# Block-causal attention ahead of two feed-forward stages: one inversion of the row sums per head, attention pipeline one to two steps deeper

## The reference

```
scores = q @ k.T / 8
scores = where(i // 64 >= j // 64, scores, -1e9)
attn = exp(scores - rowmax)
attn = attn / (attn.sum(-1) + 1e-9)
x = attn @ v                                  # 2304 x 512 after the heads are joined
x = (sigmoid(x @ w_gate) * (x @ w_val)) @ w_out      # 512 -> 1536 -> 512
p = domain_probs / (domain_probs.sum(-1) + 1e-9)
out = sum over 4 experts e of  p[:, e] * (relu(x @ w1[e]) @ w2[e])   # 512 -> 1024 -> 512
```

## Time and profile before

| | |
|---|---|
| Time, three runs | 1467.77, 1469.93, 1473.21 us (median 1469.93) |
| Profiled execution: its own time | 1468.38 us |
| its span | 1466.6 us |
| Busy over the span | PE 97%, PEld 88%, DVE 62%, ACT 50%, POOL 29% |
| Mean granted TensorE clock | 0.995 of full |

### The profile page before, as it was taken

One profiled execution on the slowest core, in us unless ns is written; L12 is line 12 of the kernel. 1 busy time (PEld: TensorE's weight loads), 2 busy tenths in 40 slices (PEclk: granted clock), 3 DMA queues, 4 the chain that ended last, 5 costly groups with the idle time before them and its releaser, 6 DMA issues.

```text
span 1466.6 us, 22252 instructions
## 1 busy us (share of the span) xinstructions
PE 1418.0 (97%) x7816; PEld 1288.6 (88%) x7816; DVE 905.8 (62%) x1557; ACT 728.5 (50%) x1472; POOL 424.0 (29%) x665
## 2 busy tenths in 40 slices
PE   6999988899999999999999999999999999999999
PEld 4777776799998989898999989899899999899897
DVE  4888879777646446376774546364857746364453
ACT  4878777666434334254663534253546535253341
POOL 3656655544302122021441112021134312021200
PEclk9999999999999999999999999999999999999999
DMA  7787797223214121122223132131222322131302
GB/s 177 182 205 179 188 225 174 60 66 87 81 35 144 44 86 59 57 87 86 65 81 100 60 100 65 51 95 45 77 87 72 98 61 72 44 101 43 97 12 79
DMA packets 201150, 136.76 MB, mean 93 GB/s; under 512 B 66096, under 2 KB 170576, under 8 KB 201040
## 3 DMA queue, kind: packets, MB, share of 16 engines
q1 hardware_dynamic: 200976, 135.31, 33.2%
q0 software_dynamic: 64, 0.04, 0.1%
HBM read 97.55 MB, written 9.44 MB: 73 GB/s over the span
## 4 chain that ended last, share of the span: by engine, by line
PE 84%; DVE 8%; DMA 2%; issue 2%; ACT 1%; SPq 1%; POOL 1%; ACTq 0%; DVEq 0%; POOLq 0%
PE pb L903 26%; PE pb L905 25%; PE pb L904 25%; PE pt L395 3%; PE ov L420 2%; DVE ptl L330 2%; DVE nmax L308 1%; PE st L432 1%; PE st L383 1%; DMA craw<-in_moe_w_dram 1%; PE st L384 1%; DVE x1p L343 1%; DMA xb<-x1d 1%; DVE qtl L336 1%; DVE ktl L336 1%
## 5 line engine op out<-in xcount | busy, mean ns | idle before, releaser
L903 PE MATMUL pb<-xch,ul 128*128 128x384 f32 x1176 | 398.9, 339 | 5.7 <-DVE cb L837 4.2
L905 PE MATMUL pb<-xch,uh 128*128 128x384 f32 x1176 | 393.5, 335 | 0.0
L904 PE MATMUL pb<-xcl,uh 128*128 128x384 f32 x1176 | 393.3, 334 | 0.0
L697 POOL TENSOR_TENSOR us<-ura 128x256 f32<-128x256 f32 x84 | 62.3, 742 | 851.4 <-DVE ul L659 833.2
L903 PEld LDWEIGHTS pb<-xch,ul 128*128 128x128 f32 x1176 | 220.7, 188 | 23.8 <-issue 16.7
L905 PE MATMUL pb<-ch,rh 128*128 128x512 f32 x576 | 224.6, 390 | 0.0
L904 PE MATMUL pb<-cl,rh 128*128 128x512 f32 x576 | 224.5, 390 | 0.0
L903 PE MATMUL pb<-ch,rl 128*128 128x512 f32 x576 | 224.0, 389 | 0.0
L904 PEld LDWEIGHTS pb<-xcl,uh 128*128 128x128 f32 x1176 | 220.9, 188 | 0.4
L905 PEld LDWEIGHTS pb<-xch,uh 128*128 128x128 f32 x1176 | 220.7, 188 | 0.0
L806 DVE TENSOR_TENSOR cl<-craw,ch 128x512 fp32r<-128x512 f32 x132 | 92.0, 710 | 114.4 <-ACT ch L741 114.0
(11 more groups left out here) (99 smaller groups left out, 2558.2 us busy)
## 6 DMA issues: line engine op xcount, KB each, us to landing
ura<-in_moe_w_dram SPq DMA_DIRECT2D x96, 256.0 KB, 3.1
craw<-in_moe_w_dram SPq DMA_DIRECT2D x96, 256.0 KB, 2.8
ura<-in_moe_w_gate_dram SPq DMA_DIRECT2D x36, 256.0 KB, 3.2
ura<-in_moe_w_val_dram SPq DMA_DIRECT2D x36, 256.0 KB, 3.2
craw<-in_moe_w_out_dram SPq DMA_DIRECT2D x36, 256.0 KB, 3.1
qhl<-qth SPq DMA_DIRECT2D x32, 144.0 KB, 2.7
qhl<-qtl SPq DMA_DIRECT2D x32, 144.0 KB, 2.6
qlh<-qtl SPq DMA_DIRECT2D x32, 144.0 KB, 2.6
```

The source lines that it names most:

```text
L697: nc.gpsimd.tensor_tensor(us[:, 0, :], a21, a22, ALU.add).then_inc(us_ok, 1)
L903: nc.tensor.matmul(acc, lhs[1], rhs[0], start=start, stop=False, skip_group_check=True)
L904: nc.tensor.matmul(acc, lhs[0], rhs[1], start=False, stop=False, skip_group_check=True)
L905: return nc.tensor.matmul(acc, lhs[0], rhs[0], start=False, stop=stop, skip_group_check=True)
```

## The change

The row sums of a head are completed and inverted once, after its fifth tile, instead of after the third and again after the fifth. Since the first tiles of a head can be normalised only then, the transpositions and the halves of them come two steps later (LAG_T 6 to 8, LAG_HI 5 to 7, LAG_LO 6 to 8), and the product with v and the output one step later (LAG_PV 13 to 14, LAG_OHI 15 to 16, LAG_OLO 16 to 17). The loop gets one more step at its end (TAIL), and from p5(1) on the products woven in at the end stand one step later.

```diff
--- before.py
+++ after.py
@@ -25,7 +25,7 @@
 
 
 STEPS = 5 * HEADS
-TAIL = 17
+TAIL = 18
 X1_RING = 2
 
 
@@ -56,9 +56,9 @@
     MASKED = -1e30
     SCALE = 1.0 / D ** 0.5
 
-    LAG_T, LAG_HI, LAG_LO, LAG_PV, LAG_OHI, LAG_OLO = 6, 5, 6, 13, 15, 16
+    LAG_T, LAG_HI, LAG_LO, LAG_PV, LAG_OHI, LAG_OLO = 8, 7, 8, 14, 16, 17
     PV_PARTS = {0: (0,), 1: (1,), 2: (2, 3, 4)}
-    INVERSE = {0: 3, 3: 5}
+    INVERSE = {0: 5}
     BODY = 20
 
     AT = [0, 256, 512, 896, 1408]
@@ -1152,18 +1152,18 @@
                 p7(0)
             if k == 6:
                 p1(1)
-            if k == 7:
+            if k == 8:
 
                 pe.wait_ge(pt_lo, 6 * HEADS)
                 p5(1)
-            if k == 8:
+            if k == 9:
                 p4(0)
                 p6(1)
-            if k == 9:
+            if k == 10:
                 p2(1)
-            if k == 10:
+            if k == 11:
                 p3(1)
-            if k == 11:
+            if k == 12:
                 p7(1)
 
         attention(nc, block, q, k, v, x1d, o_ok, x1_out, with_act, with_dve, with_pool, with_pe, with_sp)
```

## The result

The changed kernel takes 1520.95 us (median of 4 runs, 1518.31 to 1523.18), the kernel before 1471.07 beside it (1467.77 to 1473.21): 1.0342 times as long, 95% interval 1.0326 to 1.0358. That is 49.9 us more. The forecast was 31 more, 1500, in a range that ended at 1516: the sign was right and the size was not.

A forecast was written before the change was run, and what follows sets the result against it. Attention was taken as bound by a loop handed round between engines, 7.66 us a head. Terms 37 + 1 - 1 - 10 + 4 gave +31 us, so 1500 us, with an 8-in-10 range of 1481 to 1516.

The forecast's parts named there:

- loop, 26 heads: Attention, fourth head to last that makes a prep: 9.08 us a head against 7.66, +37 us.
- two heads without prep: Attention's two heads without a prep: 8.1 us against about 7.5, +1 us (0 to 3).
- side work and clock: Attention: side work partly falls into VectorE's new gaps and the `xb` wait shrinks, -10 us (-20 to 0).
- filling: Pipeline start: for two more steps TensorE has no transpositions ahead of its scores, -1 us (-3 to 0).
- end: Attention's end: leftover TensorE work and p5(1)'s wait for VectorE's last split cost together +4 us (1 to 6).
- A: From tile 0's row maximum to tile 2's: TensorE's list sets it, 3.25 us, between 3.10 and 3.4.
- B: From tile 2's row maximum to tile 3's: VectorE's work with tile 4 and the output, 2.00 us (before 0.74).
- C: From tile 3's row maximum to the next head's tile 0: same road as before, 3.83 us against 3.76.
- third rival: Attention loop: only VectorE's lists count, TensorE keeps ahead; loop 8.2 us, total 1480 us; chance 10%.
- The saving: VectorE, between tiles 3 and 4: removed completion and inversion, up to 0.46 us a head, counted at 0 (-15 to 0).
- GpSimd: Its five normalisations now in a row, later ones each needed a step later: 0 us (0 to 3).
- a rival, at 8%: Attention: TensorE's gaps lower the clock; if in every second head, +20 us, total 1520 us; chance 8%.

The follow-up runs named there:

- mends: Changed kernel with unread filler transpositions in TensorE's two waits, mixing weights in step 44 not 40, VectorE's unit 2 weight splits behind head 30's output sum: 1503.7 us.
- the tail edit: Changed kernel with VectorE's two splits of unit 2's weights at k = 8 instead of k = 7, behind the output sum of head 30: 1514.8 us.
- The experiment that moved the pair: Kernel before, with VectorE's completion and inversion for tiles 0 to 2 behind the row maximum of tile 4 instead of ahead of it: 1475.33 us.
- The kernel with earlier products: Changed kernel with product with v and output a step earlier (LAG_PV, LAG_OHI, LAG_OLO = 13, 15, 16): 1537.89 us.

## Why the prediction was right in its loop and too low in its sum

The middle is 26 heads with a prep and two without. In us of the profiled executions (the last column is the changed kernel with the three edits together, here called mends, span 1502.5; its M0 at 41.98 and 307.95):

| term | forecast | measured | with the mends |
|---|---|---|---|
| loop, 26 heads: 9.11 - 7.66 each | +37 | +37.7 | +37.7 |
| two heads without prep: 8.37 - 7.59 each, by the undisturbed one | +1 | +1.6 | +1.6 |
| side work and clock: the rest of the middle | -10 | +3.9 | -9.5 |
| filling | -1 | +3.95 | +2.6 |
| end | +4 | +6.05 | +3.5 |
| sum | +31 | +53.2 | +35.9 |

Of the 22.2 us that the sum is short, 13.9 are side work and clock, 4.95 filling, 2 the end and 1.3 the loop with the two heads.

**The loop: right.** Forecast 3.25 + 2.00 + 3.83 = 9.08; measured 3.36 + 2.11 + 3.63 = 9.10. The signs named for it are there: two gaps in VectorE instead of one (0.87 and 1.51, where some 0.8 and 2 were named), TensorE's wait for the split of tile 4, its wait for exp ahead of prep. That the sum is right to 0.02 is luck: A and B were 0.11 longer each and C 0.20 shorter. The bounds stated for this term, 34 to 43, do not follow from the ends of A either; 3.10 and 3.4 give 33 and 41. (The third rival's terms, too, make 1484 and not 1480.) One sign of being wrong came too, in the profile of the tail edit only: a granted clock under 1 in heads without side work. That two steps cost so much and one step about 0.55 shows what a lag is in a loop of five: not only a depth, but a place in each engine's list.

**The saving: right at 0.** The experiment that moved the pair, and the one that kept both inversions in the deep pipeline, show it from two sides. VectorE's 85% was no reason to count it.

**GpSimd: right at 0 in the quiet loop, and by a narrow margin.** At a lag of 6 the single inversion makes TensorE wait 45.7 us for it; at 7 the matmuls wait 5.1 us and at 8 (the changed kernel) 1.6, the weight loads ahead of them still 18.8.

**Side work: this step failed.** I took 10 us off since side work would fall into the loop's new gaps. The last column shows that it does, when the clock stays: -9.5. But side work that lands on VectorE or ScalarE also adds to TensorE's waits, and the clock fell. Six times in attention that happened, each for one to two heads, and it took back the whole credit and 4 us more. I had the fall as a rival, at 8%, and had put it aside by one row, where TensorE was busy 2.87 of 4 us and kept its clock. That row is like the quiet loop here (14.26 of 18.30 busy is 3.1 of 4, and the clock did hold), not like the heads with side work, where TensorE was busy 1.80 of 4 us ahead of the fall. The price of a fall could be read in the first row of that group (a clock of 0.63); what I had not asked is how many more there would be: six in the middle where before had two. The Trainium skill's page "TensorE: Matmul & The Clock Gate" says in "A second HAM failure mode: psum-queue depth-cycling" that frequent short pauses between groups of matmuls can make the clock swing and that the loss comes between the bursts. This trace agrees in kind: no wait of TensorE ahead of the fall at 96 was longer than 1.69 us. The quiet loop's pauses of 1.14 and 0.82 us in each head left the clock at 1.00 for 36 us (52 to 88) here, and in the profile of the tail edit it fell behind such pauses (105.60).

So the rival had the mechanism that the forecast lacked, and not its form. In this profile the falls stand in or just behind heads with side work, not in every second head. They don't come at fixed places, though: the profile of the tail edit has two of its falls in heads without any. What starts a fall stays open; that removing the step-40 job or filling the waits makes most of them go is what the runs show. The rival's sum (+20, 1520) agrees with the measured time partly by luck, because filling and end, which it took as forecast, were short by 7 us as well.

**The filling: this step failed too.** Forecast -1, measured +4.0. Five prep matmuls take 1.39 us at 27.6 and 1.41 still at 40.1; before they took 1.26 at 28.0 and 0.83 at 36.9. So the changed kernel's TensorE was still at 1.2 GHz at about 41 us, where before it had left that level by 37 us. That it has fewer transpositions to do there is a likely reason, not a tested one. With the mends, where the prep at 28.1 takes 0.86 and the one at 39.7 takes 0.91, it is still +2.6; what of the +3.95 is the clock and what the order was not separated.

**The end: near, with one term missing.** The +1.5 for `p5(1)` is the first row of TensorE's waits here, 1.28. The second I had not seen (TensorE's waits in its timeline):

```profile
346.11 0.44 PE L903 MATMUL pb<-xch,ul 128*128 128x384 f32 x1 [1.28 <-DVE ptl L330]
349.96 0.66 PE L420 MATMUL ov<-pth,vs 128*128 128x384 f32 x1 [2.54 <-DVE x1p L343]
```

VectorE's timeline shows what the output sum stood behind:

```profile
345.97 0.68 DVE L651 TENSOR_TENSOR ul<-ura,uh 128x512 fp32r<-128x512 f32 x1
347.80 1.23 DVE L659 TENSOR_TENSOR ul<-us,uh 128x1024 fp32r<-128x1024 f32 x1 [1.15 <-ACT uh L639]
349.06 0.76 DVE L343 TENSOR_TENSOR x1p<-ov,x1p 64x576 f32<-64x576 f32 x1
```

With the later lags the sum of head 30 comes behind the weight splits of the second unit, which wait 1.15 us for ScalarE. The clock is 0.71 in the window from 348 to 352. With the splits in another order the end is +3.5, near the forecast of +4.

So 18.9 us were missed between the medians (49.9 for 31). With the mends the kernel is 34.3 us above the kernel before beside it, so they take back 15.6, and what they leave is the forecast within 4 us. That side work and lost clock together made the loss in the middle is shown: with the waits filled and the step-40 job moved, 13.4 us of it go, and so do five of the six falls. How much of it is wait and how much is clock is not told apart, since each causes the other.

## What to carry to other kernels

- In a software pipeline over engines that work their lists in order, a lag also fixes where in the cycle an instruction stands. Lay out the two or three lists that hand the loop round, with start-to-start times, before adding a lag: that gave each of three parts within 0.2 us here and their sum, 9.10, within 0.02, while busy shares gave nothing.
- When a loop gets gaps in TensorE, price falls of the clock as a term of their own, first for the iterations where something else adds a wait, and take no credit for side work that "falls into the gaps" unless the clock holds there.
- One profile shows where the clock fell in one execution. A second execution of the same lists had as much clock lost, 20.4 us, at other places, so compare the sum and not a single fall.

## What the runs showed of the hardware

- Matmuls that nobody reads can keep the clock up: with 14 transpositions per head where TensorE waits, 6.9 us of clock are lost from 44 us on instead of 22.2. The quiet loop is 9.11 us as without, and the kernel 8.7 us shorter.
- The waits of one head do not tell whether the clock falls. The quiet loop, with gaps of 1.14 and 0.82 us in 9.1, kept a granted clock of 1.00 from 52 to 88 us in one profile. Behind waits of 1.69, 1.14 and 0.86 us it fell to 0.51 in that profile (100 to 104). In the profile of the tail edit the same three waits left it at 1.00, and it fell to 0.70 (104 to 108) and 0.50 (116 to 120) in heads with the quiet loop's waits alone. The kernel with earlier products, whose waits of 0.81 and 1.14 us stand 1.9 us apart (45.84 and 47.75), lost its clock in about every second head; TensorE was busy 2.05 of 4 us at 44 to 48, and the clock was 0.67 at 56 to 60, behind the next pair of such waits.
- The granted clock of the profile reads 1.00 from the start of the trace, while the durations show the lower level: in the changed kernel's profile window 16 to 20 us is at 1.00, and the prep in it (17.07) takes 1.39 us for five matmuls, which take 0.86 at full speed. The first value under 1.00 stands at 96 us, though the prep at 40.06 takes 1.41 too. At the start of a trace read durations, not the clock.
